# A mixture-of-experts router that searches six digits instead of seven, with a wider tally and another order in the tail

## The reference

```python
logits = x @ w_gate
order = np.argsort(-logits.flatten())
for idx in order:
    tok, e = int(idx) // E, int(idx) % E
    if assigned[tok] >= 0 or counts[e] >= cap:      # cap = N // E = 384
        continue
    assigned[tok] = e
    counts[e] += 1
...
for e in range(E):
    mask = assigned == e
    out[mask] = np.maximum(x[mask] @ w1[e], 0.0) @ w2[e]
```

## Time and profile before

| | |
|---|---|
| timed executions | 1332.58, 1336.51, 1332.58 us, median 1332.58 |
| profiled execution | 1322.12 us, its span 1320.4 us |
| TensorE busy | 1229.1 us (93%) |
| VectorE busy | 916.9 us (69%) |
| ScalarE busy | 574.0 us (43%) |
| mean granted clock of TensorE | 0.968 |

### The profile page before, as it was taken

One profiled execution on the slowest core, in us unless ns is written; L12 is line 12 of the kernel. 1 busy time (PEld: TensorE's weight loads), 2 busy tenths in 40 slices (PEclk: granted clock), 3 DMA queues, 4 the chain that ended last, 5 costly groups with the idle time before them and its releaser, 6 DMA issues.

```text
span 1320.4 us, 27840 instructions
## 1 busy us (share of the span) xinstructions
PE 1229.1 (93%) x9680; PEld 1093.4 (83%) x9680; DVE 916.9 (69%) x1826; ACT 574.0 (43%) x1232; POOL 287.1 (22%) x346
## 2 busy tenths in 40 slices
PE   6999983289999999999999999999999999999997
PEld 5888872277787787888898999989999899999986
DVE  4777765897887887765696666667666666666662
ACT  4666650123333233344415544545455444544541
POOL 4000000202202102120214332423233242332422
PEclk9999995589999999999999999999999999999999
DMA  8788744433332432543315233233434423334210
GB/s 147 168 169 167 165 99 176 153 112 106 128 121 64 149 127 75 177 150 121 110 34 192 66 110 112 80 104 103 128 119 127 141 79 104 100 125 135 88 43 13
DMA packets 174298, 154.65 MB, mean 117 GB/s; under 512 B 105117, under 2 KB 137885, under 8 KB 174240
## 3 DMA queue, kind: packets, MB, share of 16 engines
q1 hardware_dynamic: 151552, 102.83, 27.9%
q0 software_dynamic: 16128, 44.56, 11.1%
q10 hardware_dynamic: 6560, 6.49, 1.4%
HBM read 206.13 MB, written 33.75 MB: 182 GB/s over the span
## 4 chain that ended last, share of the span: by engine, by line
issue 37%; PE 36%; DVE 10%; POOL 9%; DMA 4%; ACT 2%; POOLq 1%; DVEq 0%; ACTq 0%
PE bank L766 8%; PE bank L786 6%; DMA out<-result,token_now 3%; PE bank L642 3%; POOL partial L421 3%; POOL out L431 3%; PE bank L651 2%; PE bank L630 2%; POOL held L401 2%; PE bank L666 2%; PE bank L1000 2%; POOL x L405 2%; PE bank L712 2%; PE bank L1027 2%; PE bank L751 1%
## 5 line engine op out<-in xcount | busy, mean ns | idle before, releaser
L569 DVE TENSOR_TENSOR w_part<-w_sb,w_part 128x1024 fp32r<-128x1024 f32 x280 | 341.7, 1224 | 104.2 <-ACT w_part L563 96.7
L563 ACT CAST w_part<-w_sb 128x1024 fp32r<-128x1024 f32 x280 | 290.5, 1046 | 206.8 <-PE bank L1027 154.4
L1000 PEld LDWEIGHTS bank<-x2T,w_part 128*128 128x128 f32 x2688 | 326.3, 192 | 3.7 <-issue 1.0
L1000 PE MATMUL bank<-x2T,w_part 128*128 128x256 f32 x2688 | 328.0, 283 | 1.1 <-DVE x2T L1557 0.6
L1027 PE MATMUL bank<-w_part,h2T 128*128 128x512 f32 x1344 | 312.6, 391 | 0.0
L1027 PEld LDWEIGHTS bank<-w_part,h2T 128*128 128x128 f32 x1344 | 250.1, 188 | 51.0
L786 PE MATMUL bank<-w_part,hT 128*128 128x512 f32 x576 | 154.9, 406 | 3.7 <-DVE w_part L569 3.7
L766 PE MATMUL bank<-xgT,w_part 128*128 128x384 f32 x768 | 146.4, 343 | 1.2 <-DVE xgT L1221 1.2
L1915 ACT ACTIVATE h2T<-bank 128x512 fp32r<-128x512 f32 x112 | 66.9, 597 | 176.8 <-PE bank L1000 176.8
L379 POOL DMA_INDIRECT xg<-x_dram,token_of x24 | 29.5, 1230 | 510.1 <-DVE token_of L1256 269.2
L766 PEld LDWEIGHTS bank<-xgT,w_part 128*128 128x128 f32 x768 | 133.6, 190 | 2.9 <-DVE xgT L1221 1.4
(11 more groups left out here) (281 smaller groups left out, 1306.7 us busy)
## 6 DMA issues: line engine op xcount, KB each, us to landing
w_sb<-in_moe_w SPq DMA_DIRECT2D x280, 512.0 KB
k_in<-in_k SPq DMA_DIRECT2D x32, 240.0 KB
v_in<-in_v SPq DMA_DIRECT2D x32, 240.0 KB
q_in<-in_q SPq DMA_DIRECT2D x32, 192.0 KB
x_dram<-x_sb SPq DMA_DIRECT2D x32, 192.0 KB, 3.0
out<-zeros SPq DMA_DIRECT2D x1, 6144.0 KB, 19.7
y_dram<-y_sb ACTq DMA_DIRECT2D x24, 256.0 KB, 2.0
x<-y_dram,slot_now POOLq DMA_INDIRECT x56, 3.6
```

The lines of the kernel that those rows point to most:

```text
L563: scalar.copy(split_part(0, c), raw_part(c)).then_inc(hi_ready[c], 1)
L569: nc.vector.tensor_tensor(split_part(1, c), raw_part(c), split_part(0, c).bitcast(F32), ALU.subtract).then_inc(lo_ready[c], 1)
L1000: last = nc.tensor.matmul(bank[2 + g % 2][:, at:at + TILE], w1_part[a][:, kt, f * P:(f + 1) * P], x2T[b][:, kt, :], start=(f % 2 == 0 and ...
```

## The change

Six digits replace seven: 6, 6, 5, 5, 5 and 5 bits, so `BINS` becomes 64, and the first two digits use 64 bins while the others use 32. The tally becomes 4 matmuls of 96 columns, whose 6 groups VectorE adds up as it reads them. The units of combine, the turns and the gates are dealt out anew over the digits. On VectorE `taken_rows(k, 1)`, `taken_tokens` and the last `s1_low` and `w_low` of j move to other digits, and `w_low(k, 3)` moves from the seventh digit to the end of the tail. On ScalarE the order is changed too.

```diff
-SHIFTS = (27, 22, 17, 12, 7, 2, 0)
-BINS = 32
+SHIFTS = (26, 20, 15, 10, 5, 0)
+BITS = (6, 6, 5, 5, 5, 5)
+BINS = 64
+    TALLY = 6
 # TensorE, step
-                before_votes = (0, 6, 9, 12, 15, 18, 22)
-                after_votes = (3, 8, 11, 14, 17, 20, 24)
+                before_votes = (0, 5, 6, 12, 15, 20)
+                after_votes = (3, 6, 10, 14, 18, 24)
                     count(n, s)
-                    if k is not None and s >= 5:
-                        turn_xg(k, 2 * (s - 5))
+                    if k is not None:
+                        if s == 2:
+                            sum_tokens(k, bank[6][:, 0:2 * TPE])
+                        if s >= 4:
+                            turn_xg(k, 2 * (s - 4))
...
                         combine(j, done, before_votes[s])
-                        if s == 6:
-                            gate_y(j, 1, k)
+                        if s == 5:
+                            turn_y(j, 1)
                     vote(n, s)
-                    if k is not None:
-                        if s == 2:
-                            sum_tokens(k, bank[6][:, 0:2 * TPE])
-                        if s >= 5:
-                            turn_xg(k, 2 * (s - 5) + 1)
+                    if k is not None and s >= 4:
+                        turn_xg(k, 2 * (s - 4) + 1)
...
                         combine(j, before_votes[s], after_votes[s])
-                        if s in (3, 5):
-                            turn_y(j, (s - 3) // 2)
-                        if s == 4:
-                            gate_y(j, 0, k)
+                        if s == 3:
+                            turn_y(j, 0)
+                        if s >= 4:
+                            gate_y(j, s - 4, k)
                 pe.wait_ge(chosen_up, n + 1)
-                for c in range(COLS):
-                    last = nc.tensor.matmul(tally_ps, ones[:], chosen[:, c, :], start=(c == 0), stop=(c == COLS - 1))
+                for c in range(0, COLS, TALLY):
+                    last = nc.tensor.matmul(tally_ps, ones[:], chosen[:, c:c + TALLY, :].rearrange("p c e -> p (c e)"),
+                                            start=(c == 0), stop=(c + TALLY == COLS))
...
                     hidden(k, 0)
+                if j is not None:
+                    gate_y(j, 2, k)
                 pe.wait_ge(tied_up, n + 1)
...
-                    hidden(k, 1)
-                if j is not None:
-                    gate_y(j, 2, k)
-                if k is not None:
-                    for f in range(2, 4):
+                    for f in range(1, 4):
                         hidden(k, f)
 # VectorE, step: before the wait for the counts of digit s
-                        if s in (1, 2):
-                            taken_rows(k, s - 1)
-                        if s == 3:
-                            taken_tokens(k, bank[6][:, 0:2 * TPE])
-                        if s == 6:
+                        if s == 1:
+                            taken_rows(k, 0)
+                        if s == 5:
                             xg_low(k, 1)
                         if s >= 3:
                             w_low(k, s - 3, 1)
+                    if j is not None and s == 2:
+                        s1_low(j, 7)
+                        w_low(j, CH + 3, 1)
...
 # VectorE, step: between met and the wait for the votes
-                        if s >= 5:
-                            xg_low(k, 2 * (s - 5))
-                    if j is not None and s == 1:
-                        s1_low(j, 7)
-                        w_low(j, CH + 3, 1)
+                        if s == 1:
+                            taken_rows(k, 1)
+                        if s == 2:
+                            taken_tokens(k, bank[6][:, 0:2 * TPE])
+                        if s >= 4:
+                            xg_low(k, 2 * (s - 4))
...
-                link(V.tensor_copy(tally[:], tally_ps))
+                link(V.tensor_reduce(tally[:], tally_ps.rearrange("p (c e) -> p e c", c=TALLY), AX.X, ALU.add))
...
                 link(V.tensor_tensor(free[:], free[:], colt[0][:], ALU.subtract))
                 if k is not None:
+                    s1_low(k, 3)
                     w_low(k, CH + 1, 1)
-                    s1_low(k, 3)
+                    w_low(k, 3, 1)
```

More of the change, by code:

```diff
@@ L715, in vote @@
             def vote(n, s):
-                bins = 4 if SHIFTS[s] == 0 else BINS
+                bins = 1 << BITS[s]
                 pe.wait_ge(met_up, n * len(SHIFTS) + s + 1)
@@ L1350, in step @@
                 for s, shift in enumerate(SHIFTS):
-                    bins = 4 if shift == 0 else BINS
+                    bins = 1 << BITS[s]
                     bits = threshold0 if s == 0 else threshold
@@ L1795, in step @@
                 if k is not None:
-                    w_high(k, 0, 1)
+                    for c in range(2):
+                        w_high(k, c, 1)
                 if j is not None:
@@ L1799, in step @@
                 if k is not None:
-                    for c in range(1, 3):
-                        w_high(k, c, 1)
+                    w_high(k, 2, 1)
                 if j is not None:
                     copy_yT(j, 0)
-                    copy_y(j, 1)
-                if k is not None:
-                    w_high(k, 3, 1)
-                if j is not None:
-                    copy_gate(j, 0)
                 if k is not None:
@@ L1812, in step @@
                 if j is not None:
-                    copy_yT(j, 1)
+                    copy_y(j, 1)
+                    copy_gate(j, 0)
                 if k is not None:
@@ L1816, in step @@
                 if j is not None:
-                    copy_gate(j, 1)
+                    copy_yT(j, 1)
                 if k is not None:
@@ L1820, in step @@
                     w_high(k, CH, 1)
+                if j is not None:
+                    copy_gate(j, 1)
+                if k is not None:
+                    w_high(k, 3, 1)
                 if j is not None:
@@ L1825, in step @@
                     s1_high(k, 0)
-                    w_high(k, CH + 1, 1)
-                    s1_high(k, 1)
                 if j is not None:
@@ L1830, in step @@
                 if k is not None:
-                    for f in range(2, 6):
+                    w_high(k, CH + 1, 1)
+                    for f in range(1, 6):
                         s1_high(k, f)
```

12 lines of the change are left out of this document (6 added, 6 removed).

## The result

The changed kernel takes 1364.36 us (median of 4, 1360.58 to 1368.24) where the kernel before takes 1333.3 (4 runs, 1332.58 to 1336.51) on the same chip: a ratio of 1.0227, 95% interval 1.0205 to 1.0248. It is slower by 31.1 us. The forecast was +24.8 and 1357.4, in a range of 1341 to 1367. The profiled execution took 1367.22, its span 1365.5. The profile that the forecast was built on took 1322.12, so from profile to profile the change is +45.1 and not +31.1; the difference between these two figures is taken up at the end.

What follows compares the result with a forecast made beforehand. The order of time at four places of a step, not busy sums, was taken as the bound. Full steps +19.2, round 6 +2.7, round 1 +3.8, round 0 -0.9 gave +24.8; 1346.9 plus 10.5 gave 1357.4 us, range 1341 to 1367.

Steps and rivals of the forecast that it cites:

- Wide digits: First two `above` cost 0.79 us more each, 64 bins free on TensorE; six uncovered digits save 0.6 us.
- Front: Start of a full step: second count at 8.3 not 7.5 us, third at 13.6 not 13.0, `met` 0.5 later.
- Round 1: Tally 0.8 us late since the turn already waited for the gather; with the end of the step, +3.8 us.
- ScalarE: After the tally, `copy_gate(1)` and `w_high(3)` stand before `copy_y(2)`; TensorE waits some 1.6 us for the turn.
- Tail: VectorE's path from last slice to next first count: 7.9 us, was 4.99; TensorE covers 4.4, waits 3.5.
- Tally: 24 matmuls in 0.77 us become 4 in some 0.3, saving 0.5; VectorE's sum costs 0.1 more.
- The full steps: Rounds 2 to 5: each step goes from 51.5 to 56.3 us, +4.8, together +19.2.
- The 10.5: Runs' median lies 10.5 us above the profiled execution; added to 1346.9 it gives 1357.4.
- rival 4: TensorE's clock falls in full steps' new waits: 0 to 3.9 us a step, 1367 at 2; chance 0.14.
- Rival 1: TensorE stays the bound in full steps and the kernel gets faster: -12 us, 1320.5; chance 0.04.
- rival 2: Front of the step and ScalarE's order cost nothing, only the step's end does: +0.8 a step, about 1341; chance 0.1.
- rival 3: ScalarE's part 3 finds its place earlier and the turn does not wait: +3.2 a step, 1350.5; chance 0.17.

Runs made afterwards that it cites:

- part 3 earlier on ScalarE: Changed kernel with `w_high(3)` moved behind `w_high(2)` on ScalarE, no longer between `copy_gate(1)` and `copy_y(2)`: 1350.7 us, ratio 1.0206 to the kernel before.
- second set: Follow-up runs on another chip, with the unchanged kernel before (median 1336.3 us) and the changed kernel again (1364.85 us, ratio 1.0217).
- third chip: Chip of a further set of follow-up runs, where the kernel before ran unchanged: median 1334.9 us, one profiled execution 1336.87 us.
- filled kernel: Changed kernel with unread matmuls on TensorE, 28 ahead of the first count and 15 ahead of the third: 1361.85 us, ratio 1.0199 to the kernel before.
- kernel filled ahead of the first count: Changed kernel with 28 unread matmuls of 256 columns on TensorE ahead of the first count in rounds 2 to 6: 1358.79 us, ratio 1.0274.
- first set: Follow-up runs on one chip, without a timing of the unmodified changed kernel; the kernel before had median 1322.5 us there.

## Why the prediction was right, and where it was off

The theory was that VectorE and ScalarE stand late at four places of a step, and that each place costs what their rows add up to. The four places came out close to what was foretold. The rival that came true beside it was the clock.

- **Wide digits.** `above` was foretold at 1.75 and took 1.76. That 64 bins are free on TensorE was wrong: 0.64 us more for each count at half clock, 0.16 at full. Round 0, foretold at -0.9, came out at 33.25 against 32.70 from first count to first count, +0.55. Its two wide counts explain 1.28 of this difference of 1.45. Six digits save nothing there: from first count to tally 20.63 us, before 20.65.
- **Front.** The third count came at 13.54 (foretold 13.6), the second at 9.11 with the clock at half and at 8.23 where it was held full (foretold 8.3). The wait on `met` is 0.5, as foretold. (The forecast's 6.05 from second to third `above` adds up to 6.12 from its own terms, which changes none of its points by 0.1.)
- **Round 1.** Foretold +3.8, measured 50.89 against 46.66, +4.2. The turn waits for the gather there, 8.1 us behind its list as before. In the step read above the list is ready at t = 16.1, as foretold, but the turn comes only at 25.85 and waits for nothing; where TensorE came earlier (part 3 earlier on ScalarE, round 3) the turn waited 0.8 for it.
- **ScalarE.** Foretold 1.6, measured 1.61 in the steps with j and k. Taking the weight part away left 0.7.
- **Ties.** Their wait is gone, as foretold.
- **Tail.** Foretold 7.9 with a wait of 3.5; measured 7.94 with 3.51 to 3.58. Taking away 1.14 and 0.79 of it took 1.1 and 0.8 off the wait, in three kernels.
- **Tally.** Foretold at 0.5 less on TensorE, measured 0.43. In a full step it is worth nothing.
- **The full steps.** 56.3 foretold, 60.3, 60.8, 57.7 and 61.0 measured, 14.7 over in the four. Of these, 2.1 lie ahead of the third count and 4.0 behind the tally; they come with the half clock. The other 8.5 lie between third count and tally (24.2 to 25.8 for 22.8), where the half clock and the late signals work together, and no run separates them in this profile. Round 6 is about 6 us longer for 2.7 foretold.
- **The sum.** +24.8 was added up on a profile of 1322.12 that shows no late signals. From that profile to this one the change is +45.1, 20.3 over the sum: 14.7 in the full steps, about 3 in round 6, 1.45 in round 0 and 0.4 in round 1. From median to median it is +31.1 (+28.6 on the chip of the second set), 6.3 over, since the median before already holds time that its profile does not.
- **The 10.5.** The forecast carried the distance of that profile from the median before over to the changed kernel, without a reason. Here the median is 2.9 below the profile. A sum too small by 20.3 and a term too large by 13.3 make the 7.0 us by which the total missed. The third chip shows what such a distance can hold: 8.7 us of late signals in four steps. If they cost both kernels alike, the term was right and the sum 6.3 short; the changed kernel was never timed on a chip without them, so this is not shown. That the total came so near is luck in this part.

What failed is the likeliest case's premise that the clock stays full: rival 4 gave its fall 0.14, and named a granted clock under 0.95 in a full step as its sign. The clock was 0.86 to 0.93 in the full steps and fell in every one, up to three times. Rival 4's price, 2 us a step at its middle, is borne out by what can be read: 2.1 to 2.8 a step where the filled kernel held the clock on the chip of the second set, and 1.7 over the forecast in each step of the kernel filled ahead of the first count, whose profile has no late signals. The path was another than rival 4's: it charged only the work ahead of the second count, which cost 0 to 1.1 a step, and had neither the fall behind the third count (12 matmuls of `combine` in 4.39 to 5.46 us for 3.02) nor that behind the turn (1.6). The measured time lies between the forecast and that rival. The Trainium skill, "TensorE: Matmul & The Clock Gate", section "HAM oscillation", says that a loop whose waits return runs the start of each pass at half rate. By that rule, the trace agrees in part: in rounds 2, 5 and 6 the first count was already at half rate, in rounds 3 and 4 it ran full (0.92) and the clock fell behind it (0.50 from 412 on). Whether such a stretch lies on the path is another matter.

Rival 1 fell at the first count of every step, rival 2 at the third count and at the turn, rival 3 at the turn's 1.61. What stays open is why VectorE resumes 1 to 2.9 us late while or just after GpSimd issues its gathers on some chips. It was seen in both kernels and not taken apart, so that the gathers are its cause is not shown.

## What to carry to other kernels

Where three engines take turns on one chain, price a change at the places where one of them is already late, by the start and the end of the single instructions, and not by busy sums: here less work on TensorE lost 2.3%, and the same work in another order gained 0.9%. Before moving a piece, list what stands behind it in its engine's queue and who waits for that; a copy that waits for another engine holds up all of it. Before a half-clock stretch is given a price, look whether a wait stands behind it that would swallow it. And when a profile and the timed median of a kernel differ by as much as the change is worth, find where the difference lies before adding it to a forecast.

## What the hardware showed that was not expected

- Weight columns: 24 matmuls of 8 moving columns take 0.80 us with 32 or 128 bf16 weight columns and 1.44 with 64, at 1.2 GHz; 0.76, 0.76 and 0.92 at 2.4.
- The granted clock fell also behind waits of 0.9 to 1.8 us, when the waits around them were long, and the fall moved to the next wait when one was filled.
- On some chips VectorE resumed 1 to 2.9 us after the matmul that it waited for had ended, at the time of the indirect gathers, and ScalarE, where it waited for TensorE too, at the same moment (432.49 and 432.54; 420.50 and 420.55). In the profiles of the first set this never happened in a full step.
- One and the same kernel had medians from 1322.5 to 1336.3 us in the sets of runs.
